# Last stage of a fused attention, experts and feed-forward kernel: whole turns held as 32-bit integers, and the cosine taken as a sine without an absolute value

## What is computed

```python
attn_out = retention(q, k, v)                 # 4 x 8 heads, 576 positions, 64 wide, decay per head
x = moe(attn_out as (2304, 512), ...)         # two of 8 experts per token, 512 -> 1024 -> 512, relu
h = x @ w_in                                  # (2304, 512) @ (512, 2048)
g = h * np.cos(h)
out = (g @ w_out).astype(np.float32)          # (2304, 2048) @ (2048, 512)
```

## Time and profile before

| | |
|---|---|
| runs | 953.77, 949.57, 948.57 us; median 949.57 us |
| span of the profiled execution, first to last instruction | 947.9 us |
| TensorE matmul busy | 933.0 us (98%) |
| TensorE weight load busy | 829.8 us (88%) |
| VectorE busy | 561.4 us (59%) |
| ScalarE busy | 531.7 us (56%) |
| granted TensorE clock, mean | 0.996 |

### The profile page before, as it was taken

How to read it: one execution, slowest core, us unless ns; L and a number is a source line. 1 busy time by engine, 2 the same in 40 slices (tenths; PEclk the granted TensorE clock), 3 DMA queues, 4 the chain that set the end, 5 groups by cost and what they waited for, 6 DMA issues and landing times.

```text
span 947.9 us, 16767 instructions
## 1 busy us (share of the span) xinstructions
PE 933.0 (98%) x5978; PEld 829.8 (88%) x5978; DVE 561.4 (59%) x1124; ACT 531.7 (56%) x965; POOL 96.3 (10%) x93
## 2 busy tenths in 40 slices
PE   8999999999999999999999999999999999999998
PEld 7989888989898888889888889888978888888887
DVE  4788646555656555533341245577777777777665
ACT  2556637645546555544441356566756765766655
POOL 2266610000000000000000232001100100000000
PEclk9999899999999999999999999999999999999999
DMA  9988657799999999975335369867656855666561
GB/s 363 329 328 280 218 149 254 187 313 321 310 302 313 308 321 288 260 221 157 106 103 216 100 232 320 306 250 285 232 192 257 293 208 193 240 235 236 205 236 56
DMA packets 113113, 230.44 MB, mean 243 GB/s; under 512 B 47384, under 2 KB 71640, under 8 KB 104856
## 3 DMA queue, kind: packets, MB, share of 16 engines
q1 hardware_dynamic: 107288, 210.73, 67.1%
q0 software_dynamic: 5760, 18.88, 5.5%
HBM read 157.65 MB, written 61.70 MB: 231 GB/s over the span
## 4 chain that ended last, share of the span: by engine, by line
PE 81%; DVE 7%; ACT 7%; issue 3%; DMA 2%; POOL 0%; SPq 0%; DVEq 0%; ACTq 0%
PE ps L1781 18%; PE ps L1763 17%; PE ps L1951 14%; PE ps L1937 12%; PE ps L1801 3%; PE ps L1878 3%; PE ps L1866 3%; PE ps L1815 2%; PE ps L1687 2%; ACT angle L1044 2%; PE ps L1710 2%; PE ps L1702 2%; PE ps L1735 2%; DVE angle L1546 1%; ACT angle L1042 1%
## 5 line engine op out<-in xcount | busy, mean ns | idle before, releaser
L1951 PE MATMUL ps<-w_sb,g_hi 128*128 128x512 f32 x576 | 180.6, 395 | 0.9 <-DVE g_lo L1551 0.8
L1763 PE MATMUL ps<-xs,w_hi 128*128 (+1 forms) x784 | 173.2, 303 | 0.0
L1763 PEld LDWEIGHTS ps<-xs,w_hi 128*128 128x128 f32 x784 | 131.2, 188 | 3.4 <-issue 0.5
L1374 DVE TENSOR_TENSOR w_lo<-raw,w_hi 128x1024 fp32r<-128x1024 f32 x48 | 58.8, 1226 | 123.1 <-ACT w_hi L877 123.1
L1937 PE MATMUL ps<-x_odd,w_sb 128*128 128x320 f32 x672 | 117.7, 310 | 2.6 <-DVE h_sb L1531 1.2
L1937 PEld LDWEIGHTS ps<-x_odd,w_sb 128*128 128x128 f32 x672 | 106.0, 188 | 15.1 <-issue 3.1
L1763 PE MATMUL ps<-xs,w_lo 128*128 (+1 forms) x392 | 118.7, 303 | 0.0
L877 ACT ACTIVATE w_hi<-raw 128x1024 fp32r<-128x1024 f32 x48 | 50.9, 1060 | 117.2 <-PE ps L1781 117.2
L1951 PE MATMUL ps<-w_sb,g_lo 128*128 128x512 f32 x288 | 112.4, 390 | 0.0
L1951 PEld LDWEIGHTS ps<-w_sb,g_hi 128*128 128x128 f32 x576 | 100.8, 188 | 11.3 <-issue 1.7
L1781 PE MATMUL ps<-w_hi,hs_lo 128*128 128x512 f32 (+1 forms) x245 | 96.7, 395 | 0.0
(11 more groups left out here) (200 smaller groups left out, 1615.0 us busy)
## 6 DMA issues: line engine op xcount, KB each, us to landing
w_sb<-w_pairs SPq DMA_DIRECT2D x24, 1792.0 KB, 7.9
w_sb<-w_pairs SPq DMA_DIRECT2D x40, 1024.0 KB, 9.5
raw<-weights SPq DMA_DIRECT2D x64, 512.0 KB, 4.7
w_pairs<-stage SPq DMA_DIRECT2D x24, 1024.0 KB, 7.6
qk<-qk SPq DMA_DIRECT2D x18, 512.0 KB, 6.9
kv<-kv SPq DMA_DIRECT2D x18, 512.0 KB, 5.9
y_slots<-zeros_sb SPq DMA_DIRECT2D x33, 256.0 KB
raw_pair<-pairs SPq DMA_DIRECT2D x8, 1024.0 KB, 8.8
```

The costliest lines, as they stand in the source:

```text
L1374: tt(w_lo[:, at], raw[:, f % 2, :], w_hi[:, at].bitcast(F32), ALU.subtract).then_inc(split_done, 1)
L1763: last_one = nc.tensor.matmul(ps[5 + half][:, 0:HALF], w[:, at:at + P], xs[:, bass.ds(g % 2, 1), a, k, half * HALF:(half + 1) * HALF].rear ...
L1951: last_one = nc.tensor.matmul(ps[j][:, :], a[:, slot % 2, part, j * C:(j + 1) * C], w2_sb[slot % 3][:, hl, part * DM:(part + 1) * DM], sta ...
```

## The change

In `turn`, the tile `turns` becomes a tile of 32-bit integers, and the bias is minus a quarter: `turns` is the whole number that the write makes of `h - 0.25`. `reduce` reads that tile and adds 0.0 in place of minus ROUND. `angle` then lies between -0.75 and 0.25, and 2 pi angle + pi/2 between -pi and pi, where `Sin` gives the cosine directly. The absolute value and the wait on its own semaphore are gone: ScalarE has 112 instructions fewer (16 of 384 columns and 96 of 320). No other instruction moves on any engine, and the number of table loads on ScalarE (12) and their places are the same.

```diff
@@ -86,6 +86,7 @@
+QUARTER = 0.25
@@ -183,7 +184,7 @@
-            turns = [keep(f"turns{i}", [P, TB], F32, st) for i in range(2)]
+            turns = [keep(f"turns{i}", [P, TB], I32, st) for i in range(2)]
@@ -301,7 +302,7 @@
-        turn_done, angle_done, abs_done, sin_done = sem("turn_done"), sem("angle_done"), sem("abs_done"), sem("sin_done")
+        turn_done, angle_done, sin_done = sem("turn_done"), sem("angle_done"), sem("sin_done")
@@ -1033,15 +1034,13 @@
-                nc.scalar.activation(turns[c % 2][:, 0:n], h[:, 0:n], ACT.Copy, bias=ROUND).then_inc(turn_done, 1)
+                nc.scalar.activation(turns[c % 2][:, 0:n], h[:, 0:n], ACT.Copy, bias=-QUARTER).then_inc(turn_done, 1)
 
             def cosine(slot, q):
                 c = chains_before(slot) + q
                 a = angle[c % 4][:, 0:width(slot)]
                 act.wait_ge(angle_done, c + 1)
-                nc.scalar.activation(a, a, ACT.Abs).then_inc(abs_done, 1)
-                act.wait_ge(abs_done, c + 1)
-                nc.scalar.activation(a, a, ACT.Sin, scale=-2.0 * np.pi, bias=tab("half_pi")).then_inc(sin_done, 1)
+                nc.scalar.activation(a, a, ACT.Sin, scale=TURN, bias=tab("half_pi")).then_inc(sin_done, 1)
@@ -1537,7 +1536,7 @@
-                stt(angle[c % 4][:, 0:n], turns[c % 2][:, 0:n], -ROUND, h_of(slot, q)[:, 0:n], ALU.add, ALU.subtract
+                stt(angle[c % 4][:, 0:n], turns[c % 2][:, 0:n], 0.0, h_of(slot, q)[:, 0:n], ALU.add, ALU.subtract
                     ).then_inc(angle_done, 1)
```

## The result

| | before | changed |
|---|---|---|
| median of the runs, us | 950.67 (4 runs, 948.57 to 953.77) | 940.78 (4 runs, 940.39 to 943.99) |
| ratio, 95% interval | | 0.9904 (0.9887 to 0.9922) |
| span of the profiled execution, us | 947.9 | 938.6 |
| ScalarE busy, us | 531.7 | 482.3 |
| matmul busy, us | 933.0 | 927.2 |

The change makes the kernel 0.96% faster, 9.9 us between the medians and 9.3 us between the profiled executions. The forecast was 941.1 us in a range from 939.5 to 945.8.

The account below looks back on a forecast made before the run. TensorE bounds the kernel, losing 9.08 us in last-stage slots where VectorE's drains come late. Less 0.6 us left unsaved, 8.5 us off the 949.57 us median gave 941.1 us, range 939.5 to 945.8 us.

Parts of the forecast that it names:

- The list of lost stretches: Last stage: turns of the slot loop longer than turns without a hole lose 9.08 us of TensorE time.
- slots 7 to 9: Last stage: 0.83, 1.45 and 0.94 us lost; six absolute values in the chain of waits offer 3.3 us with gaps.
- The two changes of block: Slots 13 to 16 and the same four of the next block: 2.81 and 2.84 us lost, counted as gained whole.
- Slot 17: A turn of 13.73 us against a floor of 13.52 us; 0.21 us lost, counted as gained whole.
- The chain, 0.50 us each: From reduce to product, each chain gets 0.50 us shorter, so product waits that much less for the sine.
- drain 3: VectorE in slot 13: 1.3 us late behind three absolute values; without them it starts as soon as its product is there.
- The 0.6 us left unsaved: Slots 7 to 9: 0.6 us withheld from the gain, because slot 9 looked tight, with output and gathered rows in both lists.
- the first rival: Late stretches: VectorE's own list sets drains, so each stretch gains 0.50 us once; 5.4 us, 944.2 us; chance 0.20.
- Integers at nothing: turn and reduce: integer write and read taken at the float forms' price, 468 and 489 ns, so no cost.
- dearer integers: turn and reduce: integers cost 0.10 us more on each, leaving about 6 us gain, 943.6 us; chance 0.08.
- half speed: turn and reduce: conversion doubles both, each chain 0.46 us longer, kernel slower by 10 us, 959.6 us; chance 0.05.
- other waits set the holes: TensorE's holes: set by inputs or banks the chain does not touch, so nothing comes back, 949.6 us; chance 0.07.

Follow-up runs that it names:

- The copy behind the sine: Changed kernel with a copy of the integer tile onto itself after each sine, 112 in all; median 941.60 us, ratio 0.9897 to the kernel before.

## Why the prediction was right

**What bounds the kernel.** The list of lost stretches was nearly the whole of it. Line by line: slots 7 to 9 were to give 0.83 + 1.45 + 0.94 = 3.22 us. From the load at 611.17 us to the one at 639.73 us the kernel before took 28.56 us, and the changed one takes 25.30 us (610.90 to 636.20 us), 3.26 us less. (Slot 8, from first product to first product, takes 10.67 us now, so its floor was 0.11 us lower than the 10.78 us that I had worked out.) The two changes of block were to give 2.81 and 2.84 us, and gave 55.54 - 52.73 = 2.81 and 55.57 - 52.73 = 2.84 us. Slot 17 was to give 0.21 and gave 0.22 us. That is 9.13 of the 9.4 us by which the stage is shorter; the rest, 0.3 us, lies in two places that I had not listed. From the first product of the stage to the first step of the second product it took 6.56 us (547.66 to 554.22 us) and takes 6.34 us now (547.78 to 554.12 us); and the last half of slot 6 took 4.27 us (600.41 to 604.68 us) and takes 4.18 us now (600.23 to 604.41 us).

**Length and not idle time.** TensorE's matmul busy time was a poor guide to what could be gained. The Trainium skill says so of it as a measure of how close a kernel is to roofline, because pipelined instructions look smaller in the trace (Perfetto Trace Analysis, Identifying the Most-Contended Engine). This case agrees that it misleads, but the other way: the 293 matmuls of the first change of block are busy for 54.32 us before and for 52.73 us after. The records were longer where TensorE waited (product 6 of slot 13 has 1.15 us, product 3, without a wait, 1.04 us), and so the idle time hid half of the loss. By idle time no more than 4.65 us could have come from these stretches; 9.13 us came. The slots without a hole gave the floor to a hundredth of a microsecond.

**The chain, 0.50 us each.** In slot 13 drain 3 was to come as soon as its product is there, and it comes 0.10 us behind. Drain 4 was to be 1.3 us earlier and is 1.23 us earlier in its slot. VectorE's `product` waits for the sine 63 times and 29.0 us in all, where it had been 87 times and 62.9 us. That is 0.30 us less for each of the 112 chains, and not the 0.5 us that I named as a sign: 25 chains had no such wait to lose, and product 1 of slot 13, for one, had waited for 0.34 us only. The copy behind the sine shows that latency is the cause, and the runs with the absolute value in chosen slots show where.

**The 0.6 us left unsaved** is the one term of the sum that was clearly off. I kept it for slot 9, where 3.3 us on offer stood against 3.22 us; nothing was lost there. Where the larger margin came from was not tested. The 9.4 us measured in the stage are 0.9 us above the 8.5 us forecast: the 0.6 us, and 0.3 us from the places not listed. That the median of 940.78 us comes within 0.4 us of the 941.1 us forecast is in part luck. The forecast started from a median before of 949.57 us; with one more run that is 950.67 us, and from there the same 8.5 us would give 942.2 us. The high end of the range, by the terms named for it (944.2 us for the first rival and 1 us for the median), comes to 945.2 us and not 945.8; nothing hangs on it.

**Integers at nothing.** Right: 472 and 492 ns, and the kernel with integers alone is as the kernel before. With that the rivals of dearer integers and of half speed fall. The rival in which each late stretch gains 0.50 us once (5.4 us) falls by the windows: each change of block gave back 2.8 us, where it would have given 1.84 us. The rival that other waits set the holes falls too: no wait of a matmul is left in this stage.

## What to carry to other kernels

Where one engine is the bound and others feed it in a loop, measure a turn of the loop that has no hole, and take the other turns' lengths less this floor as what can be gained; the engine's idle time can show half of it. Then count how many instructions of a kind lie one behind the other on the way round: taken off the chain, an instruction is worth its latency as many times as it stands there, until the feeding loop is shorter than the bound, and nothing after that. So it was here: three absolute values stood ahead of drain 3 of slot 13, which now starts 1.24 us earlier in its slot (7.49 us behind the load, where it was 8.73 us), and in the last block, where TensorE had no hole, they were worth nothing. Placed where nobody waited for it, an instruction of about the same length (457 ns against 470) cost nothing.

## What I had not expected

One more absolute value costs five times what the first did: 0 of them 390.8 us, 1 of them 400.2 us, 2 of them 448.7 us for the last stage. I had expected 10 to 18 us for the second, by counting three in a round, where all four chains of a slot stand in line once VectorE has no backlog to work on meanwhile.
